# Attention and two dense layers on one core: head 0's keys loaded and rotated alone, zeros multiplied in two pauses

## What is computed

```python
def rotate(x):
    x1, x2 = (x[..., :half], x[..., half:])
    return np.concatenate([x1 * cos - x2 * sin, x1 * sin + x2 * cos], axis=-1)
q_rot, k_rot = (rotate(q), rotate(k))
scores = scale * np.matmul(q_rot, k_rot.transpose(0, 1, 3, 2))
scores = scores - np.max(scores, axis=-1, keepdims=True)
attn = np.exp(scores)
attn = attn / (np.sum(attn, axis=-1, keepdims=True) + 1e-09)
x = np.matmul(attn, v)                      # then (B * S, H * D)
h = x @ moe_w_in;   x = (h * sigmoid(h)) @ moe_w_out
h = x @ moe2_w_in;  y = where(h > 0, h, exp(min(h, 0)) - 1) @ moe2_w_out
```

## Time and profile before

| | us |
|---|---|
| median of the runs | 551.55 |
| the profiled run | 551.5 |
| its span | 549.5 |
| PE busy | 539.4 |
| ACT busy | 372.6 |
| POOL busy | 346.2 |
| DVE busy | 288.1 |

### The profile page before, as it was taken

One profiled execution on the slowest core, in us unless ns is written; L12 is line 12 of the kernel. 1 busy time (PEld: TensorE's weight loads), 2 busy tenths in 40 slices (PEclk: granted clock), 3 DMA queues, 4 the chain that ended last, 5 costly groups with the idle time before them and its releaser, 6 DMA issues.

```text
span 549.5 us, 9477 instructions
## 1 busy us (share of the span) xinstructions
PE 539.4 (98%) x3275; PEld 528.8 (96%) x3275; DVE 288.1 (52%) x587; ACT 372.6 (68%) x765; POOL 346.2 (63%) x277
## 2 busy tenths in 40 slices
PE   7899999999999999999999999999999999999997
PEld 7788899999999999999999999999999999999997
DVE  5788865743368853436663347784244430067400
ACT  3889878866578966658886568886566653356531
POOL 5988989759747646646655654445455666556662
PEclk9899999999999999999999999999999999999999
DMA  8676655666455455443443333333333443444440
GB/s 322 206 210 195 176 182 146 183 202 185 118 168 167 125 150 178 129 128 130 125 129 127 117 111 106 117 114 115 113 115 127 130 135 119 131 120 129 135 143 29
DMA packets 45790, 79.52 MB, mean 145 GB/s; under 512 B 6832, under 2 KB 14384, under 8 KB 45744
## 3 DMA queue, kind: packets, MB, share of 16 engines
q1 hardware_dynamic: 44016, 76.57, 46.0%
q10 hardware_dynamic: 1728, 2.36, 1.2%
HBM read 63.57 MB, written 2.36 MB: 120 GB/s over the span
## 4 chain that ended last, share of the span: by engine, by line
PE 91%; ACT 4%; DMA 1%; issue 1%; POOL 1%; SPq 1%; DVE 0%; ACTq 0%; POOLq 0%
PE banks L1166 72%; PE banks L1067 5%; PE banks L1044 3%; PE banks L1050 3%; PE banks L1127 3%; PE banks L1120 2%; ACT prob L561 1%; DMA k_raw<-k 1%; PE banks L1080 1%; PE banks L1102 1%; ACT pt L575 1%; POOL k_raw L391 0%; ACT v_st L552 0%; PE banks L1129 0%; PE banks L1122 0%
## 5 line engine op out<-in xcount | busy, mean ns | idle before, releaser
L441 POOL TENSOR_TENSOR w_lo<-w_raw,w_hi 128x512 fp32r<-128x512 f32 x192 | 247.5, 1292 | 184.5 <-ACT w_hi L627 182.9
L627 ACT CAST w_hi<-w_raw 128x512 fp32r<-128x512 f32 x189 | 116.9, 622 | 33.5 <-PE banks L1166 30.7
L1166 PE MATMUL banks<-x_lo,w_hi 128*128 128x384 f32 x384 | 128.8, 335 | 0.1
L1166 PE MATMUL banks<-g_lo,w_hi 128*128 128x384 f32 x384 | 128.6, 335 | 0.0
L1166 PE MATMUL banks<-x_hi,w_lo 128*128 128x384 f32 x384 | 128.5, 335 | 0.0
L1166 PE MATMUL banks<-g_hi,w_hi 128*128 128x384 f32 x384 | 128.4, 334 | 0.0
L1166 PE MATMUL banks<-g_hi,w_lo 128*128 128x384 f32 x384 | 128.4, 334 | 0.0
L1166 PE MATMUL banks<-x_hi,w_hi 128*128 128x384 f32 x384 | 128.4, 334 | 0.0
L765 DVE TENSOR_REDUCE neg_max<-banks 128x1 f32<-128x576 f32 x72 | 54.2, 754 | 54.9 <-PE banks L1050 53.7
L639 ACT ACTIVATE act_buf<-banks 128x384 f32<-128x384 f32 x96 | 47.3, 493 | 41.4 <-PE banks L1166 40.7
L1166 PEld LDWEIGHTS banks<-x_lo,w_hi 128*128 128x128 f32 x384 | 72.1, 188 | 1.0 <-issue 0.8
(11 more groups left out here) (112 smaller groups left out, 707.0 us busy)
## 6 DMA issues: line engine op xcount, KB each, us to landing
w_raw<-w SPq DMA_DIRECT2D x192, 256.0 KB, 2.6
q_raw<-q SPq DMA_DIRECT2D x11, 384.0 KB, 3.9
q_one<-q_raw SPq DMA_DIRECT2D x44, 96.0 KB, 2.7
k_raw<-k SPq DMA_DIRECT2D x7, 576.0 KB, 5.5
k_st<-k_raw SPq DMA_DIRECT2D x28, 144.0 KB, 2.5
v_raw<-v SPq DMA_DIRECT2D x8, 320.0 KB, 3.7
out<-act_buf ACTq DMA_DIRECT2D x12, 192.0 KB, 2.6
k_both<-k_st SPq DMA_DIRECT2D x15, 144.0 KB, 3.0
```

Source lines behind the costliest of these rows:

```text
L441: nc.gpsimd.tensor_tensor(w_st[LO][:, slot, :], w_raw[:, slot, :], w_st[HI][:, slot, :].bitcast(F32), ALU.subtract).then_inc(w_lo_done, 1)
L627: nc.scalar.copy(w_st[HI][:, slot, :], w_raw[:, slot, :]).then_inc(w_hi_done, 1)
L1166: last = nc.tensor.matmul(dst, w_st[wp][:, slot, m * P:(m + 1) * P], src[xp][:, tile, :], start=start and n == 0, stop=stop and n == 2)
```

## The change

1. **Loads.** Keys 0 are loaded in three requests: both halves of the lower 64 partitions (head 0) where the whole halves stood, and the upper 64 partitions (head 1) with both halves in one request behind queries 0.
2. **Rotation of the first pair.** POOL multiplies head 0's keys, queries 0, and then head 1's keys, before it starts on queries 1. DVE rotates head 0's keys, then queries 0, makes head 0's low parts, then rotates head 1's keys (`first_keys_rope(1)`), and takes max(0) and max(1). The low parts of head 1's queries and keys follow behind max(1).
3. **ACT.** Head 1's first high part stands behind the queries' high parts. `queries_hi(1)` moves behind the cast of T(0), `keys_hi(1)` behind exp(2) and ahead of the cast of T(1), `values_hi(0)` behind exp(3).
4. **Placing.** `place_q_one` waits for the queries' high part alone; `place_keys` is cut in two, and the keys' high part is copied before the queries' low part. `load_keys(2)` waits for both heads' adds.
5. **Zeros.** The first block is 22 + 2 + 3 + 3 instead of 30 + 4 + 3 + 2 + 2; nine follow S(1) (into bank 4) and four follow the end transposes of tiles 0 and 1 (into `pv_out`).

```diff
             def load_keys(r):
                 if r == 2:
-                    sp.wait_ge(first_k_roped, 1)
+                    sp.wait_ge(first_k_roped, 2)
...
             def place_q_one(r, par):
-                sp.wait_ge(q_lo_done, r)
+                sp.wait_ge(q_hi_done, r)
...
-            def place_keys(r, par):
-                i, ready = 2 * r + par, k_placed[par]
-                rows, others = rows_of[par], other_rows_of[par]
+            def place_keys_hi(r, par):
+                i, rows = 2 * r + par, rows_of[par]
+                sp.wait_ge(k_hi_done, r)
+                sp.wait_ge(scored, QN * (i - 1))
+                sp.dma_start(k_st[rows, i % SLOTS, :].bitcast(F32), k_raw[r % 2][rows, 1, :]).then_inc(k_placed[par], 16)
+
+            def place_keys_lo(r, par):
+                i, rows, others = 2 * r + par, rows_of[par], other_rows_of[par]
                 sp.wait_ge(k_lo_done, r)
                 sp.wait_ge(scored, QN * (i - 1))
...
             def place(r, par):
                 place_q_one(r, par)
+                place_keys_hi(r, par)
                 place_q_two(r, par)
-                place_keys(r, par)
+                place_keys_lo(r, par)
...
-            sp.dma_start(k_raw[0][:, 0, :], k[0:P, 0:S]).then_inc(k_first_in, 16)
+            sp.dma_start(k_raw[0][lower, 0, :], k[0:D, 0:S]).then_inc(k_first_in, 16)
             sp.dma_start(table[:, 1, :], rope[:, S:2 * S]).then_inc(sin_in, 16)
-            sp.dma_start(k_raw[0][:, 1, :], k[0:P, S:2 * S]).then_inc(k_in[0], 16)
+            sp.dma_start(k_raw[0][lower, 1, :], k[0:D, S:2 * S]).then_inc(k_second_in, 16)
             sp.dma_start(q_raw[0][:, 0, :], q[0:P, 0:CT]).then_inc(q_first_in, 16)
             sp.dma_start(q_raw[0][:, 1, :], q[0:P, CT:2 * CT]).then_inc(q_in[0], 16)
+            sp.dma_start(k_raw[0][upper, :, :], k[D:P, :].rearrange("p (a n) -> p a n", a=2)).then_inc(k_in[0], 16)
...
-            nc.gpsimd.tensor_tensor(k_raw[0][:, 0, :], k_raw[0][:, 0, :], table[:, 0, :], ALU.mult) \
-                .then_inc(first_k_scaled, 1)
+            nc.gpsimd.tensor_tensor(k_raw[0][lower, 0, :], k_raw[0][lower, 0, :], table[lower, 0, :], ALU.mult) \
+                .then_inc(pool_scaled, 1)
             pool.wait_ge(q_first_in, 16)
...
+            pool.wait_ge(k_in[0], 16)
+            pool.wait_ge(pool_scaled, 2)
+            nc.gpsimd.tensor_tensor(k_raw[0][upper, 0, :], k_raw[0][upper, 0, :], table[upper, 0, :], ALU.mult) \
+                .then_inc(pool_scaled, 1)
...
-            for par in range(2):
-                first_keys_hi(par)
+            first_keys_hi(0)
             for par in range(2):
                 first_queries_hi(par)
+            first_keys_hi(1)
             for n in range(H * QN):
                 exp_tile(n)
+                if n == 2:
+                    keys_hi(1)
+                if n == 3:
+                    values_hi(0)
...
+                if n == 1:
+                    queries_hi(1)
-                if i % 2 == 0:
+                if i % 2 == 0 and i:
...
+            def first_keys_rope(par):
+                rows = rows_of[par]
+                keys = first_keys[rows, :, :]
+                nc.vector.tensor_tensor(keys, halves(k_raw[0][rows, 1, :]), halves(table[rows, 1, :]), ALU.mult) \
+                    .then_inc(first_k_scaled[par], 1)
+                dve.wait_ge(pool_scaled, 2 * par + 1)
+                dve.wait_ge(first_k_scaled[par], 1)
+                nc.vector.tensor_tensor(keys, keys, halves(k_raw[0][rows, 0, :]), ALU.add).then_inc(first_k_roped, 1)
...
-            for par in range(2):
-                first_keys_lo(par)
-                first_queries_lo(par)
+            first_keys_lo(0)
+            first_queries_lo(0)
+            dve.wait_ge(k_in[0], 16)
+            first_keys_rope(1)
             max_tile(0)
             for n in range(H * QN):
                 if n < H * QN - 1:
                     max_tile(n + 1)
+                if n == 0:
+                    first_queries_lo(1)
+                    first_keys_lo(1)
...
-            zeros(30)
-            pe.wait_ge(first_k_roped, 1)
-            zeros(4)
+            zeros(22, mlp(0))
             pe.wait_ge(first_k_hi, 1)
-            zeros(3)
-            pe.wait_ge(first_k_hi, 2)
-            zeros(2)
+            zeros(2, mlp(0))
+            pe.wait_ge(first_q_roped, 1)
+            zeros(3, mlp(0))
             pe.wait_ge(first_q_hi, 1)
-            zeros(2)
+            zeros(3, mlp(0))
             score_tile(0)
             score_tile(1)
+            zeros(9, banks[:, 4, 0:CT])
...
+                if n == 1:
+                    zeros(4, pv_out)
```

More of the change, by code:

```diff
@@ L177, in build @@
         cos_in, sin_in, k_table_in = sem("cos_in"), sem("sin_in"), sem("k_table_in")
-        k_first_in, q_first_in = sem("k_first_in"), sem("q_first_in")
+        k_first_in, k_second_in, q_first_in = sem("k_first_in"), sem("k_second_in"), sem("q_first_in")
         k_in = [sem("k_in0"), sem("k_in1")]
@@ L187, in build @@
         k_roped, q_roped = sem("k_roped"), sem("q_roped")
-        first_k_scaled, first_q_scaled = sem("first_k_scaled"), sem("first_q_scaled")
+        first_k_scaled, first_q_scaled = [sem("first_k_scaled_a"), sem("first_k_scaled_b")], sem("first_q_scaled")
+        pool_scaled = sem("pool_scaled")
         first_k_roped, first_q_roped = sem("first_k_roped"), sem("first_q_roped")
@@ L272, in place_q_two, with place_keys @@
                     sp.dma_start(q_two[par][rows, 0:CT].bitcast(F32), q_lo).then_inc(ready, 16)
-            def place_keys(r, par):
-                i, ready = 2 * r + par, k_placed[par]
-                rows, others = rows_of[par], other_rows_of[par]
+            def place_keys_hi(r, par):
[5 more added lines that the diff above has]
+                i, rows, others = 2 * r + par, rows_of[par], other_rows_of[par]
                 sp.wait_ge(k_lo_done, r)
                 sp.wait_ge(scored, QN * (i - 1))
-                sp.dma_start(k_st[rows, i % SLOTS, :].bitcast(F32), k_raw[r % 2][rows, 1, :]).then_inc(ready, 16)
-                sp.dma_start(k_st[others, i % SLOTS, :].bitcast(F32), k_raw[r % 2][rows, 0, :]).then_inc(ready, 16)
+                sp.dma_start(k_st[others, i % SLOTS, :].bitcast(F32), k_raw[r % 2][rows, 0, :]).then_inc(k_placed[par], 16)
+            def place_keys(r, par):
+                place_keys_hi(r, par)
+                place_keys_lo(r, par)
             def place_both(i):
@@ L529, in first_keys_hi @@
                 rows = rows_of[par]
-                act.wait_ge(first_k_roped, 1)
+                act.wait_ge(first_k_roped, par + 1)
                 nc.scalar.mul(halves(k_st[rows, par, :]), first_keys[rows, :, :], SCALE).then_inc(first_k_hi, 1)
@@ L918, in _ @@
             dve.wait_ge(sin_in, 16)
[L919 to L924, removed]
+            dve.wait_ge(k_second_in, 16)
+            first_keys_rope(0)
             dve.wait_ge(q_in[0], 16)
@@ L927, in _ @@
                 .then_inc(first_q_scaled, 1)
-            dve.wait_ge(first_q_scaled, 2)
+            dve.wait_ge(pool_scaled, 2)
+            dve.wait_ge(first_q_scaled, 1)
             nc.vector.tensor_tensor(first_queries, first_queries, q_raw[0][:, 0, :], ALU.add) \
                 .then_inc(first_q_roped, 1)
-            for par in range(2):
-                first_keys_lo(par)
-                first_queries_lo(par)
+            first_keys_lo(0)
+            first_queries_lo(0)
+            dve.wait_ge(k_in[0], 16)
+            first_keys_rope(1)
             max_tile(0)
@@ L1201, in _, with zeros @@
             pe.wait_ge(zeros_set, 1)
-            def zeros(count):
+            def zeros(count, dst):
                 for m in range(count):
-                    nc.tensor.matmul(mlp(0), g[LO][:, FT - 1, 0:P], g[LO][:, FT - 1, :], start=m == 0,
-                                     stop=m == count - 1)
-            zeros(30)
-            pe.wait_ge(first_k_roped, 1)
-            zeros(4)
+                    nc.tensor.matmul(dst, g[LO][:, FT - 1, 0:P], g[LO][:, FT - 1, :], start=m == 0, stop=m == count - 1)
+            zeros(22, mlp(0))
             pe.wait_ge(first_k_hi, 1)
-            zeros(3)
-            pe.wait_ge(first_k_hi, 2)
-            zeros(2)
+            zeros(2, mlp(0))
+            pe.wait_ge(first_q_roped, 1)
+            zeros(3, mlp(0))
             pe.wait_ge(first_q_hi, 1)
-            zeros(2)
+            zeros(3, mlp(0))
             pe.wait_ge(ident_ready, 1)
```

5 lines of the change are left out of this document (3 added, 2 removed).

## The result

| | before | after |
|---|---|---|
| median of the runs, us | 551.39 (7 runs, 551.2 to 552.64) | 555.45 (7 runs, 553.29 to 556.75) |
| ratio to before | | 1.0065, 95% interval 1.0052 to 1.0078 |
| profiled run, us | 551.5 | 556.59 |
| its span, us | 549.5 | 554.8 |

The change makes the kernel slower by 3.6 to 4.1 us. That is above the range of the prediction (550.5 to 553.2) and more than twice the 1.65 us by which the prediction told a change from none. The direction of its likeliest case was right, its size (+0.6) far too small.

What follows compares the result with a forecast made beforehand. PE's dense-layer products bound the kernel (72% of the chain); the change only shifts the opening. Loads and first head -0.2, head 1's product and later keys +0.5 to +1.1, placing and clock -0.3: +0.6, 552.1 us; range 550.5 to 553.2.

Steps and rivals of the forecast that it cites:

- its likeliest case: Whole kernel: T(6) 0.6 us later, 552.1 us in all; chance 0.45, its own range 551.7 to 552.6.
- The loads: Opening loads: 64 partitions run at 226 GB/s, head 0's keys land at 6.37, keys 1 at 12.74 instead of 11.68.
- I save 2 x 0.12 us: Head 0's keys loads: each half takes 0.65 us instead of 0.77, so they land 0.24 us earlier.
- the upper keys take 1.30 us: Load behind queries 0: upper keys land at 8.66, everything behind them 1.06 us later.
- The early head: Opening: head 0, rotated first, lets S(0) start 0.2 us earlier, near 10.6.
- DVE against POOL: Opening: head 1's DVE product, asking at 10.44, meets POOL's queries 1; if POOL is first, exp(0) starts at 14.15, not 12.83.
- POOL and the high part of keys 1: ACT waits for POOL's keys 1, done at 17.0 or 17.9; exp(3) starts 0.5 to 0.7 us later, 18.85 to 19.05.
- I count on the fall being gone: PE's granted clock: added zeros prevent its fall at 19.3 us, worth an estimated 0.3 us.
- Rival (4): Opening: clock falls to 1.2 GHz, exp(3) 1.1 us later than forecast; +1.7, 553.2 us; chance 0.12.
- Placing: Copies for S(6): with high parts copied earlier, the low part lands at 22.4, before T(4) ends; cost 0.
- The yardstick: T(6), ending the opening at 25.9 us: what it moves by, the end moves by.
- Rivals (1) and (2): Loads of 64 partitions at full rate: 551.2 us, chance 0.2; also SBUF free for head 1's DVE product: 550.6, chance 0.1.

Runs made afterwards that it cites:

- b_dummy64: The kernel before plus one unused 442 KB load over the upper 64 partitions behind queries 0; 555.19 us, ratio 1.0055.
- a_no_pause_zeros: The changed kernel without the nine zeros behind S(1) and the four behind the end transposes; 554.85 us, ratio 1.0054.
- a_onemult: a_whole_onepool with DVE's product of both heads' keys in one operation, the two adds staying apart; 551.87 us, ratio 0.9997.
- a_whole_onepool: a_whole with POOL's product of keys 0 over all 128 partitions in one operation; 553.38 us, ratio 1.0018.
- a_whole: The changed kernel with keys 0 loaded in whole halves again, in the order of before; 552.73 us, ratio 1.0014.
- b_place: The kernel before with the change's placing alone (queries' and keys' high parts copied earlier); 552.5 us, ratio 1.0004.

## Why the prediction was wrong

**The loads** were the right step with the wrong size. The split does put the loads at half rate, and everything behind the upper keys later; but the forecast had the upper keys at 8.66 and they landed at 10.51. Two terms failed. "I save 2 x 0.12 us" at head 0's keys: they landed 0.69 later instead of 0.24 earlier. No gain is to be seen, but the loss is not shown to be the split's: 7.30 lies within the 6.40 to 7.46 of whole halves, and the 6.61 that the forecast started from is among the earliest of them. And, the larger one, "the upper keys take 1.30 us": they landed 2.8 us after the first half of the queries (7.74), where the forecast had 1.8. The windows from 7 to 10 us hold 201 to 207 GB/s, not 226, and for three microseconds; so requests beside the upper keys, too, ran at that rate. The rate in b_dummy64 (210 to 230) confirms the half, not the three microseconds; in a_no_pause_zeros, whose loads are the same, the upper keys landed at 9.98, half a microsecond earlier.

**The early head.** S(0) came at 11.57 against 10.83 before; the forecast had 10.6. All that the change could win stood in this one term, and it did not come. Here too the kernel before is an early one: a_onemult and a_whole_onepool, with whole loads, have 11.34 and 11.28.

**DVE against POOL** was right as a rule, with another partner. Head 1's product asked at 11.42, not 10.44, and waited for POOL's product of the upper keys, not for that of queries 1; it ended at 11.94, the time that the forecast had for the other, and DVE's at 12.57, 0.63 later. exp(0) came at 14.28 (14.15 forecast), exp(2) at 17.19 (17.0). These two agree by luck: the later loads and a shorter wait cancel. That rotating by heads doubles DVE's product and add, 1.5 us on the way to max(0), stood in the working, but not as what it is, the price of the change when the loads gain nothing; a_onemult shows it.

**POOL and the high part of keys 1** was the meeting place, as forecast: 19.46 instead of 17.0, by 1.85 for the landing, 0.35 for POOL's product of queries 1 behind DVE's (2.19 instead of 1.84), the rest small gaps. exp(3) came at 20.54, not 18.85.

**The clock.** "I count on the fall being gone" failed. It came at 23 us instead of 19, and stayed to 29.9, twice as long. The term was thought to be worth 0.3 us; T(3) to T(6) took 9.0 us where I had 6.8 (19.7 to 26.5), so 2.2 us were lost there. a_whole and a_onemult, with the same order of work and no fall in that stretch, took 6.7. In this run the nine value products, on the path, lay in the fall (2.29 us instead of 1.55), where before it had hit tiles that DVE and ACT hid. Nor was there much to win: of the 89 runs of the kernel before that the experiments bring, 78 have a mean clock of 1.000, so the fall at 19 us in the one profiled run was the exception. The seven runs of the changed kernel agree that a longer fall costs: those with a mean granted clock of 0.994 took 554.36 to 556.75, mean 555.9, those with 0.997 took 553.29 to 555.45, mean 554.4. Rival (4), the clock low in the opening, was seen in a_whole and in a_no_pause_zeros, not in the changed kernel's profiled run, and in a_no_pause_zeros it cost max(0) 0.3 us, not the 1.7 of the forecast.

**Placing** cost nothing and gained nothing that b_place's interval shows, as said.

**The yardstick.** "What T(6) moves by, the end moves by, since nothing after it has slack of its own": 4.8 at T(6), 5.3 at the end, and in the table up to 3.2 us more at the end than at T(6). The sentence forgot that work with slack can be overtaken. The keys' copies for S(18) (the changed kernel) or S(24) (b_place), and x_lo, cost PE no wait in the kernel before; after a shift they did.

**The sum.** Of 4.1 us by the medians, 2.7 to 3.2 go with the loads (a_whole); the remaining 0.9 to 1.4 with DVE's doubled rotation (a_onemult). Both shares hold whatever the clock did in these kernels, and how much that is stays open. The steps of the prediction that failed are, then, the upper keys' 1.30 us (2.8 measured), the 0.24 us saved at head 0 (none to be seen) and the clock's fall counted as gone (2.2 us lost in it). Rivals (1) and (2), full rate for half the partitions, are refuted by b_dummy64.

The Trainium skill, SBUF — State Buffer, section "Door 1: The DMA port swizzle", has either half of the partitions reach 8 of the 16 ports. b_dummy64 agrees, 210 to 230 GB/s against 417 to 436, and I had kept 0.3 of the chances for the other side.

## What to carry to other kernels

Do not split a load by partitions to get one half early: at half the rate (210 to 230 against 417 to 436 GB/s) half the partitions take about as long as all of them, and each request wants its own issue (0.43 us or more). A split by columns was no better here (2.3 us over before). The time of an operation on DVE and POOL does not shrink with its partitions either (576 columns: 0.76 us for 64, 0.77 for 128 on DVE, 1.40 and 1.41 on POOL); to do a tile in two halves of partitions is to do it twice. One profiled run is one draw: the same loads landed up to 1.06 us apart, so read a difference in a landing only beside several runs. When a shift in the opening of a kernel is priced, carry it past the first stage: list what stands within a microsecond of a collision (two SBUF readers on DVE beside POOL, copies that land just in time, a fall of PE's clock) and price each of them once in the range.

## What I had not expected of the hardware

A POOL operation and a DVE operation with two SBUF inputs exclude each other for whole operations: x_lo, 0.54 us of work, took up to 3.05 us. The wait can be read off: DVE ends 0.42 us after POOL for 384 columns and 0.63 for 576. SP's first eight issues took 0.38 to 0.44 us in the kernel before; of those of the changed kernel six took 0.47 to 0.59, three of them loads over all partitions that had not changed. A copy of 147 KB within SBUF, 2.5 us from issue to landing in the median before, took 4.34 at 48.5 us of the changed kernel; why stays open.
